# A fused attention and two-MLP kernel on one core: transposes moved in front of the next group's scores, weighted sums moved a batch later

## The reference

```python
# attention over chunks of 32 queries; each sees 8 memory keys and 56 keys around it
scores = scale * np.matmul(q_c, k_full.transpose(0, 1, 3, 2))
scores = scores - np.max(scores, axis=-1, keepdims=True)
a = np.exp(scores)
a = a / (np.sum(a, axis=-1, keepdims=True) + 1e-09)
out[:, :, c_start:c_end] = np.matmul(a, v_full)      # 4 x 8 x 768 x 64
...
x = out.transpose(0, 2, 1, 3).reshape(3072, 512)
h = np.maximum(np.maximum(x @ w1, x @ w2), x @ w3)   # 512 -> 768
y = h @ w_out                                        # 768 -> 512
...
h = y @ w_in                                         # 512 -> 2048
g = np.where(h >= 1, h, np.where(h <= -1, 0.0, (h + 1) ** 2 / 4))
z = g @ w_out2                                       # 2048 -> 512
```

## Time and profile before

| what | value |
|---|---|
| median of three runs | 987.39 us (986.23 to 987.53) |
| the profiled execution's own time | 987.29 us |
| its span | 985.4 us |
| PE busy | 969.7 us, 98% of the span |
| DVE, ACT, POOL busy | 470.4, 354.4, 150.1 us |
| chain of waits, share of the span | PE 98%, DVE 1%, ACT 1% |
| transposes, line 441 | 96 instructions, 15.9 us busy |
| scores, line 434 | 1536 instructions, 21.9 us busy |
| weighted sums, line 458 | 1536 instructions, 29.9 us busy |

### The profile page before, as it was taken

One profiled execution on the slowest core, in us unless ns is written; L12 is line 12 of the kernel. 1 busy time (PEld: TensorE's weight loads), 2 busy tenths in 40 slices (PEclk: granted clock), 3 DMA queues, 4 the chain that ended last, 5 costly groups with the idle time before them and its releaser, 6 DMA issues.

```text
span 985.4 us, 18546 instructions
## 1 busy us (share of the span) xinstructions
PE 969.7 (98%) x7968; PEld 905.5 (92%) x7968; DVE 470.4 (48%) x713; ACT 354.4 (36%) x553; POOL 150.1 (15%) x176
## 2 busy tenths in 40 slices
PE   5999999999999999999999999999999999999998
PEld 4999999999999999999988988899888898888897
DVE  4572514334242433425456655566545666454452
ACT  3341222222122222222344535544354544444253
POOL 1103352315225231000000000000000000000000
PEclk9999999999999999999999999999999999999999
DMA  9453643635555461042736566655656545574532
GB/s 372 174 196 106 247 184 138 252 123 194 183 214 177 178 230 61 1 171 65 259 130 206 205 236 209 208 192 200 248 185 243 192 160 195 188 258 172 192 118 107
DMA packets 32206, 181.52 MB, mean 184 GB/s; under 512 B 3456, under 2 KB 7552, under 8 KB 21888
## 3 DMA queue, kind: packets, MB, share of 16 engines
q0 software_dynamic: 9216, 92.28, 26.8%
q1 hardware_dynamic: 22912, 88.09, 24.3%
HBM read 144.70 MB, written 35.65 MB: 183 GB/s over the span
## 4 chain that ended last, share of the span: by engine, by line
PE 98%; DVE 1%; ACT 1%; DMA 0%; issue 0%
PE mlp L465 23%; PE mlp L466 23%; PE mlp L467 23%; PE attn_ps L467 3%; PE attn_ps L466 3%; PE attn_ps L465 3%; PE scores_ps L467 3%; PE scores_ps L466 3%; PE scores_ps L465 3%; PE attn_ps L458 3%; PE scores_ps L434 2%; PE trans_ps L467 1%; PE trans_ps L466 1%; PE trans_ps L465 1%; PE trans_ps L441 1%; DMA qk_raw<-qk_l 0%
## 5 line engine op out<-in xcount | busy, mean ns | idle before, releaser
L465 PE MATMUL mlp<-x_hi,w_hi 128*128 128x384 f32 x576 | 197.5, 343 | 1.6 <-issue 1.6
L467 PE MATMUL mlp<-x_lo,w_hi 128*128 128x384 f32 x576 | 193.6, 336 | 0.0
L466 PE MATMUL mlp<-x_hi,w_lo 128*128 128x384 f32 x576 | 193.3, 336 | 0.0
L466 PE MATMUL mlp<-yc,wi 128*128 128x384 f32 x448 | 150.7, 336 | 0.0
L467 PE MATMUL mlp<-yc,wi 128*128 128x384 f32 x448 | 149.6, 334 | 0.0
L465 PE MATMUL mlp<-yc,wi 128*128 128x384 f32 x448 | 149.6, 334 | 0.0
L747 ACT ACTIVATE ramp<-up,half_col 128x768 f32<-128x768 f32 x64 | 60.1, 939 | 197.4 <-DVE up L961 178.3
L465 PEld LDWEIGHTS mlp<-x_hi,w_hi 128*128 128x128 f32 x576 | 108.8, 189 | 3.7 <-issue 1.9
L466 PEld LDWEIGHTS mlp<-x_hi,w_lo 128*128 128x128 f32 x576 | 108.9, 189 | 0.0
L467 PEld LDWEIGHTS mlp<-x_lo,w_hi 128*128 128x128 f32 x576 | 108.7, 189 | 0.0
L466 PEld LDWEIGHTS mlp<-yc,wi 128*128 128x128 f32 x448 | 84.1, 188 | 8.8
(11 more groups left out here) (111 smaller groups left out, 1644.8 us busy)
## 6 DMA issues: line engine op xcount, KB each, us to landing
wi<-wi_scratch POOLq DMA_DIRECT2D x32, 1792.0 KB, 7.6
wo<-wo_scratch POOLq DMA_DIRECT2D x32, 1024.0 KB, 5.1
qk_raw<-qk_l SPq DMA_DIRECT2D x24, 768.0 KB, 8.2
wi_scratch<-stage_a SPq DMA_DIRECT2D x8, 1792.0 KB, 8.0
v_raw<-v_l SPq DMA_DIRECT2D x24, 512.0 KB, 4.8
wo_scratch<-stage_a SPq DMA_DIRECT2D x8, 1024.0 KB, 6.6
y_scratch<-y_stage SPq DMA_DIRECT2D x32, 192.0 KB, 2.5
y_raw<-y_scratch SPq DMA_DIRECT2D x8, 768.0 KB, 5.4
```

Of the source, the lines that this page charges most:

```text
L465: pe.matmul(out_ap, a_hi, b_hi, start=first, stop=False, skip_group_check=beside)
L466: pe.matmul(out_ap, a_lo, b_hi, start=False, stop=False, skip_group_check=beside)
L467: return pe.matmul(out_ap, a_hi, b_lo, start=False, stop=last, skip_group_check=beside)
```

## The change

On TensorE, in tiles 0 to 6: the transposes of group j move from the middle of block 2j + 1 to the start of block 2j + 2, in front of `scores(j+1)`. The weighted sum of group 0 moves from the start of block 2 to the start of block 4, in front of the transposes of group 1. The weighted sum of group 1 moves from the start of block 4 to the end of the first layer, in front of the transposes of group 2. The weighted sum of group 2 moves from between the layers to the middle of the second layer, behind its second call. The function `ahead` goes: the waits stand directly in front of their pieces. ACT and DVE move their `transposed`, `x_high` and `x_low` to follow. No instruction of arithmetic is added or removed.

```diff
                     j, r = divmod(f, 2)
-                    def ahead():
-                        weights_ready(n0 + j, j, t + 1)
-                        if j + 1 < GPT:
-                            scores_ready(n0 + j + 1, j + 1, t + 1)
...
                     if attention and r == 0 and j:
-                        weighted_v(j - 1)
+                        if j == 2:
+                            weights_ready(n0, 0, t + 1)
+                            weighted_v(0)
+                        transposes(n0 + j - 1, (a + j) % 2)
+                        scores_ready(n0 + j, j, t + 1)
                         scores(j)
...
                         scores(0)
-                    if attention and r:
-                        transposes(n0 + j, (a + 1 + j) % 2)
                     layer1(t, a, f, 1)
-                    layer1(t, a, f, 2, ahead if attention and r else None)
+                    layer1(t, a, f, 2)
                 if attention:
-                    weighted_v(GPT - 1)
+                    weights_ready(n0 + 1, 1, t + 1)
+                    weighted_v(1)
+                    transposes(n0 + 2, (a + 1 + 2) % 2)
                 if t < TILES - 1:
                     for d in range(KD):
                         layer2(t, a, d)
+                        if attention and d == 1:
+                            weights_ready(n0 + 2, 2, t + 1)
+                            weighted_v(2)
...
+                    if f == 4:
+                        x_high(n0, 1 - a, 0)
                     if r == 0 and j:
-                        x_high(n0 + j - 1, 1 - a, j - 1)
+                        transposed(n0 + j - 1)
                     h_first(t, a, f)
                     if r == 0:
                         exponent(n0 + j, (a + 1 + j) % 2)
-                    else:
-                        transposed(n0 + j)
...
                 h_high(t, KF1 - 1)
-                x_high(n0 + GPT - 1, 1 - a, GPT - 1)
+                x_high(n0 + 1, 1 - a, 1)
+                transposed(n0 + 2)
                 for d in range(KD):
                     y_out(t, d)
+                    if d == 1:
+                        x_high(n0 + 2, 1 - a, 2)
...
-                    if r == 0 and j:
-                        x_low(n0 + j - 1, 1 - a, j - 1)
+                    if f == 4:
+                        x_low(n0, 1 - a, 0)
...
-                x_low(n0 + GPT - 1, 1 - a, GPT - 1)
+                x_low(n0 + 1, 1 - a, 1)
+                x_low(n0 + 2, 1 - a, 2)
```

## The result

The changed kernel takes 988.53 us (median of 22 runs, 987.72 to 988.99). The kernel before takes 986.67 us in the 22 runs beside it (986.21 to 988.06). That is 1.86 us more, a ratio of 1.0016 with a 95% interval of 1.0010 to 1.0022. The forecast of 989.8 us stood on the first three runs of the kernel before, 987.39 us, and meant a rise of 2.4 us. The loss is real, and just short of the 2.0 us that the prediction took as its border.

A forecast was written before the change was run, and what follows sets the result against it. PE, busy throughout each first-half tile, was taken as the bound; its pieces rise from 7.705 to 8.045 us per tile, 0.34 more, +2.4 us in seven tiles: 987.39 + 2.4 = 989.8 us, range 988.0 to 991.6.

The forecast's parts named there:

- the 2.0 us that the prediction took as its border: About 0.2% of the time, roughly what a measurement of this kernel can tell from no change.
- e: Joint from the last transpose to the first small matmul of the scores: put at 0.21 us, between 0.11 and 0.27.
- u: Extra time from first to second transpose when small matmuls stand in front: put at 0.08 us, between 0.06 and 0.11.
- the prediction's measure: A piece's cost: start of the large product in front to start of the second one behind, less 0.345 us.
- 2e + 2u - 0.24: Loss per tile from the two unseen joints: 0.10 us at their low ends, 0.52 at the high; 0.34 forecast.
- slower by over 0.2%: Outcome of the whole kernel losing more than about 2.0 us, given chance 0.62.
- same: Outcome of the whole kernel staying within about 0.2%, 2.0 us, given chance 0.33.
- rival 1: Joints at the transposes are cheap, e near 0.15 and u near 0.06: +1.3 us, 988.7 us; chance 0.29.
- Rival 2: Each interruption of large products has a fixed toll whatever its shape; joining saves 2.9 us, 984.5 us; chance 0.06.
- Rival 3: Satisfied waits in front of small matmuls stop their feed: up to +5.9 us on top, 993 to 995; chance 0.06.
- Rival 4: Late y loads make DVE hold `h_third` back and PE wait: a few us, 992 us; chance 0.02.
- Cost nothing: Verdict on the later last `x_low` and y loads: y lands near 435.5 us, its use moves to about 438.

The follow-up runs named there:

- the case above: The kernel before with only the last weighted sum moved, behind the second call of the second layer: 988.06 us, ratio 1.0008.

## Why the prediction was right, and where it was off

**What bounds the kernel: right.** PE fills every tile, before and after. The effect is what PE's pieces cost beside their neighbours.

**The pieces: right, to 0.03 us.** Block 2 was put at 1.435 us and is 1.435; block 4 at 2.67 and is 2.645; sum and transposes at 1.68 and are 1.665. The cost of entering scores behind transposes, e, was put at 0.21 and is 0.20. The extra on the first transposes, u, was put at 0.08 and is 0.06, which is the row at the lower clock.

**The size of the loss was put too high**: 0.34 us per tile forecast, 0.26 measured. The term that was off most is u, 0.02 too high in two places; e was 0.01 too high in two. With the measured values the prediction's own formula, 2e + 2u - 0.24, gives 0.28. The rest lies where the prediction's measure does not reach, behind the second product. There the next two products behind a lone T start 0.176 and 0.182 us after their forerunner instead of 0.173, so a lone T costs about 0.01 more than its 0.445, and three of them per tile went away.

**The time.** The result is 1.3 us under the forecast. Of that, 0.5 us is the loss (2.4 forecast, 1.9 measured), and 0.7 us is the base: three runs of the kernel before gave 987.39 us, 22 gave 986.67. The range held the time, and the direction was right. The chance of "slower by over 0.2%" (0.62) stood on a loss that was too high: at 0.16% to 0.19% the result stands in the case "same", halfway between the forecast and rival 1.

**The rivals.** Rival 1 (cheap joints) was right on u, 0.06, and wrong on e, which is 0.20 and not 0.15. Rival 2 (a fixed toll) is wrong: block 2 came to 1.435 us and not 1.23, block 4 to 2.645 and not 2.30, and the order inside a piece counts by 0.16 to 0.20 us. Rival 3 (the waits) is wrong: with the waits early, the distances are the same to 0.01 us. Rival 4 (the loads) is wrong, and the profile's list of waits shows PE waiting for DVE only once behind the start, in the second half, as before:

```profile
PE mlp L465 <- DVE g_hl L979: 0.3, 1, 0.3
```

**What was overlooked.** "Cost nothing" for moving the last sum was true only because the change put another sum and transposes between the layers. Moved alone, it uncovers two waits of PE for DVE.

**The rule on modes.** The Trainium skill, "TensorEngine Tiling (Array Packing)", Key Properties, says that a change of tiling mode drains TensorE. By its count of changes alone the loss was +1.4 us; with the slow second product behind small matmuls and the prediction's u, +2.4; measured +1.86. The trace agrees with the rule in that entering small matmuls costs 0.09 to 0.10 us, from transposes as from large products; it does not show what happens in that time. It is not the whole of it: leaving costs 0.11 more on the second large product, but only 0.06 on the second transpose. With sum and scores parted there are two changes more per tile, as in the changed kernel, and the loss is 0.41 us against 0.26, so the count of changes alone does not give the time.

## What to carry to other kernels

Where PE is full, as here, read the timeline from start to start around each interruption, and price an order by its joints: which pieces of small matmuls are neighbours, and which shape stands on the side where PE leaves the small matmuls. Whole-array transposes beside whole-array products cost nothing at the joint here, and they were cheapest behind small matmuls: 2.445 us behind sum and scores, 2.485 in front, 2.645 between them. And before a piece is moved away from a place, ask what its time there was hiding.

## What the runs showed of the hardware

- A sum with the transposes right behind it is cheaper than both apart: 1.665 against 1.275 + 0.445 = 1.72 us. Behind the sum the second transpose starts 0.06 us late, where the second large product starts 0.11 late.
- The rise of the clock moves by itself. In front of the first scores of tile 0 the large products start 0.32 us apart, behind them 0.17 to 0.18. That is the step from the lower level (1.2 GHz) to the upper (2.4 GHz), read from the pace, since the granted clock of the profile stands at 1.00 in both stretches. The scores between them took 1.19 us in the profile before and 0.96 us in that of the changed kernel, with the same instructions in front of them:

```profile
28.99 1.19 PE L434 MATMUL scores_ps<-qk_raw 64*32 64x64 f32 x64
```

```profile
28.93 0.96 PE L434 MATMUL scores_ps<-qk_raw 64*32 64x64 f32 x64
```

The next large product started 0.29 us earlier for it (30.11 and 29.82), and the one behind it 0.45 us earlier (30.54 and 30.09). In the ten profiles, block 0 of tile 0 lasts from 8.86 to 9.86 us. That is why the spans of the two profiles differ by 1.4 us and the medians by 1.86: one profile each says less than the tiles or the medians.
- `h_low` on DVE, 0.56 us at the median, took up to 1.57 us in the kernel before and 1.43 us in the case above, where it overlapped with POOL's work on SBUF. All nine `h_low` over 0.6 us in the kernel before overlap with such work, and so do the seven in the kernel with the last sum late. But three and six others overlap with it for 0.25 us or more and take 0.56. That POOL is the cause was not tried. The Trainium skill, "VectorE: DVE Perf Modes", Two Vector instructions with no wait between them, says that the second SBUF read interface of VectorE is shared with GpSimd; the overlap agrees with it, and no run here shows more.
